# Three operations of an attention stage issued earlier in their step: the sum broadcast on TensorE, its copy on ScalarE, the main normalisation on VectorE

## The reference

```python
scores = q @ k.T / 8
scores = where(scores >= max(scores) - tau, scores, -1e9)
attn = exp(scores - max(scores)); attn /= attn.sum() + 1e-9
x = attn @ v                          # 2304 tokens x 512
h = relu(x @ w_in); x = (h * h) @ w_out
# then: 8 experts, each token goes to the best of x @ w_gate,
# relu(x @ w1[e]) @ w2[e], times its gate and a sigmoid
```

## Time and profile before

| | us |
|---|---|
| median of 3 runs | 1021.32 (1021.19 to 1021.54) |
| the profiled execution's own time | 1021.32 |
| its span, first to last instruction | 1019.6 |
| attention stage, of that | to about 317.6 |

### The profile page before, as it was taken

The page is one execution under the profiler, slowest core; times in us unless marked ns, Lnnn a source line. Parts: engine busy times, 40 slices in busy tenths (PEclk is TensorE's granted clock), DMA queues, the critical chain, the costliest instruction groups (busy, mean ns, idle before and its releaser), DMA issues.

```text
span 1019.6 us, 19281 instructions
## 1 busy us (share of the span) xinstructions
PE 994.8 (98%) x6731; PEld 828.7 (81%) x6731; DVE 627.0 (61%) x1220; ACT 585.8 (57%) x922; POOL 418.3 (41%) x725
## 2 busy tenths in 40 slices
PE   7999999999998999999999999999999999999996
PEld 5888888888886888888888888889978888888884
DVE  5888888888885334322322232235787777777773
ACT  4888787787774333322322232233548888888883
POOL 4777778778783000000000000000008866666763
PEclk9999999999999999999999999999999999999999
DMA  4322322322213110010011001005389157351110
GB/s 115 80 61 71 86 55 71 87 61 69 59 30 95 42 52 1 21 42 21 1 42 42 0 21 42 22 1 161 124 328 401 49 196 283 116 197 41 34 41 34
DMA packets 85385, 84.04 MB, mean 82 GB/s; under 512 B 49711, under 2 KB 64559, under 8 KB 85298
## 3 DMA queue, kind: packets, MB, share of 16 engines
q1 hardware_dynamic: 81778, 72.41, 23.9%
q0 software_dynamic: 3520, 10.49, 3.0%
HBM read 69.24 MB, written 15.21 MB: 83 GB/s over the span
## 4 chain that ended last, share of the span: by engine, by line
PE 66%; DVE 1%; SPq 0%; issue 0%; ACT 0%; DMA 0%; POOL 0%; ACTq 0%; POOLq 0%; DVEq 0%
PE y_ps L1167 19%; PE h_ps L1150 19%; PE y_ps L1231 16%; PE row_ps L1231 8%; PE h_ps L1262 2%; PE row_ps L1136 2%; PE y_ps L1221 1%; SPq L969 0%; SPq L965 0%; DMA y_rows<-r_buf 0%; DVE g_lo L1488 0%; ACT r_buf L1335 0%; PE h_ps L1136 0%; POOL out_dram L1058 0%; DVE y_row L1701 0%
## 5 line engine op out<-in xcount | busy, mean ns | idle before, releaser
L1483 DVE TENSOR_TENSOR g_buf<-r_buf 128x512 f32<-128x512 f32 (+1 forms) x80 | 51.1, 638 | 220.5 <-ACT r_buf L1335 219.8
L1335 ACT ACTIVATE r_buf<-h_ps 128x512 f32<-128x512 f32 (+1 forms) x80 | 44.4, 555 | 234.1 <-PE h_ps L1150 231.9
L951 POOL TENSOR_TENSOR w_lo<-w_experts,w_hi 128x2048 fp32r<-128x2048 f32 x20 | 126.2, 6309 | 73.9 <-ACT w_hi L1394 73.7
L1394 ACT ACTIVATE w_hi<-w_experts 128x2048 fp32r (+1 forms) x100 | 150.4, 1564 | 0.5 <-PE row_ps L1231 0.5
L1069 POOL MEMSET ones<- 128x128 bf16 x1 | 0.2, 210 | 356.9 <-DVE x_lo L1469 356.9
L477 ACT ACTIVATE e_sb<-s_sb,stats,live 128x576 f32<-128x576 f32 x144 | 124.5, 865 | 37.8 <-POOL stats L265 36.5
L951 DVE TENSOR_TENSOR w_lo<-w_experts,w_hi 128x1024 fp32r<-128x1024 f32 (+1 forms) x80 | 137.0, 1754 | 5.3 <-ACT w_hi L1394 5.0
L1150 PE MATMUL h_ps<-x_hi,w_in_hi 128*128 128x512 f32 (+1 forms) x320 | 119.9, 375 | 2.3 <-DVE x_lo L1469 2.3
L1167 PE MATMUL y_ps<-g_hi,w_out_hi 128*128 128x512 f32 (+1 forms) x320 | 118.0, 369 | 0.9 <-DVE g_lo L1488 0.9
L1150 PE MATMUL h_ps<-x_hi,w_in_lo 128*128 128x512 f32 (+1 forms) x320 | 117.9, 368 | 0.0
L1150 PE MATMUL h_ps<-x_lo,w_in_hi 128*128 128x512 f32 (+1 forms) x320 | 117.8, 368 | 0.0
(11 more groups left out here) (251 smaller groups left out, 2217.8 us busy)
## 6 DMA issues: line engine op xcount, KB each, us to landing
w_experts<-in_moe_w_dram SPq DMA_DIRECT2D x18, 2048.0 KB, 13.9
y_rows<-y_row SPq DMA_DIRECT2D x36, 128.0 KB, 2.4
k_raw<-in_k_dram SPq DMA_DIRECT2D x32, 128.0 KB, 3.1
q_raw<-in_q_dram SPq DMA_DIRECT2D x32, 128.0 KB, 2.9
w_raw<-in_moe_w_in_dram SPq DMA_DIRECT2D x16, 256.0 KB, 3.2
v_nat<-in_v_dram SPq DMA_DIRECT2D x16, 256.0 KB, 2.6
y_T<-in_moe_w_out_dram SPq DMA_DIRECT2D x16, 256.0 KB, 2.7
y_early<-y_row SPq DMA_DIRECT2D x32, 128.0 KB, 2.4
```

What stands on the lines that cost most here:

```text
L951: alu.tensor_tensor(group_of(w_lo, g)[:, c0:c1], raw_group(buf, g)[:, c0:c1], group_of(w_hi, g)[:, c0:c1].bitcast(F32), ALU.subtract).then ...
L1394: nc.scalar.activation(group_of(w_hi, g)[:, c0:c1], raw_group(buf, g)[:, c0:c1], ACT.Copy).then_inc(hi_done, 1)
L1483: V.tensor_tensor(g_buf[:, 0:cols], r_buf[:, 0:cols], r_buf[:, 0:cols], ALU.mult).then_inc(sq_done, 1)
```

## The change

Nothing is added or removed. In three loops a call is put further up in its step. On PE, in step `5i+1`, `broadcast_rinv(i-1)` comes ahead of the two sets of tail transposes of pair `i-1`. On ACT, in the same step, `copy_rinv(i-1)` comes ahead of their two copies. On DVE, in step `5i+2`, `normalise_main(i-1)` comes ahead of the two masks of step `5i+1`.

```diff
@@ block.tensor
+                if c == 1 and i >= 1:
+                    broadcast_rinv(i - 1)
                 if 0 <= made[0] < PAIRS:
                     for s in range(2):
                         transposed_probs(*made, s)
-                if c == 1 and i >= 1:
-                    broadcast_rinv(i - 1)
@@ block.scalar
+                if c == 1 and i >= 1:
+                    copy_rinv(i - 1)
                 if 0 <= made[0] < PAIRS:
                     for s in range(2):
                         evacuate(*made, s)
-                if c == 1 and i >= 1:
-                    copy_rinv(i - 1)
@@ block.vector
+                if c == 2 and i >= 1:
+                    normalise_main(i - 1)
                 if c == 3 and i >= 1:
                     normalise_tail(i - 1)
                 if 0 <= before[0] < PAIRS:
                     for h in heads_in(before[1]):
                         mask(*before, h)
-                if c == 2 and i >= 1:
-                    normalise_main(i - 1)
```

## The result

| | before | after |
|---|---|---|
| median of 4 runs, us | 1021.43 | 1029.14 |
| lowest to highest | 1021.19 to 1022.22 | 1028.88 to 1029.41 |
| profiled execution, its span | 1021.32, 1019.6 | 1030.98, 1029.3 |

The ratio is 1.0075, with a 95% interval of 1.0056 to 1.0092: slower by 7.7 us, against a forecast of 6.4.

A forecast was written before the change was run, and what follows sets the result against it. PE was taken to bound attention. Second-mask waits 4.40, broadcast waits 2.73 in short pairs and -0.28 in long ones, and the emptying -0.45 gave +6.40 us on 1021.32: 1027.7 us, range 1022.5 to 1031.5.

The forecast's parts named there:

- PE sets the pace, long and short pairs differ by one stall: Attention: PE's lateness is paid for; long pairs stall about 0.43 us in step 5i, behind ACT's copy.
- The mask's wait, 14 x 0.31: Step 5i+3: PE's second transpose set waits for DVE's later second mask; 4.40 us with 0.06 in the last pair.
- The broadcast's wait, 0.39 in short pairs: Step 5i+1: PE's broadcast waits for k's low part; 2.73 us over seven short pairs, -0.28 over seven long.
- The bound of 0.47: Upper limit for the short pairs' broadcast delay, if PE's release costs 0.08 more, as an accumulator read takes.
- The last pair waits for nothing at the broadcast: Pair 15 has no next k, so PE's moved broadcast has no wait there.
- ACT's order costs nothing: Step 5i+1: ACT does the same three operations, already waits 0.33 us for PE, ends equally behind it; 0.
- The emptying gains 0.45: Behind the last pair, the broadcast fills PE's idle gap before the last tail block; -0.45 us.
- The sum: Whole kernel: 4.40 + 2.73 - 0.28 - 0.45 = +6.40 us, 1027.7.
- The lost race with POOL: Rival: a POOL operation runs first and moves both masks by 0.25 us; 3.5 more, 1031.2; chance 0.15.
- The faster case: Rival: earlier POOL work lets ACT run ahead, long pairs' stall goes, masks meet PE; -3.5 us, 1017.9; chance 0.06.

The follow-up runs named there:

- e4_split: The kernel before, but POOL splits a pair's fourth weight piece behind the bias of step 5i+4 instead of ahead of it: 1017.16 us, ratio 0.9952.
- e2_normalise: The kernel before with only the change's DVE edit, the main normalisation ahead of the two masks: 1023.24 us, ratio 1.0010.
- e3_between: The kernel before with the broadcast between the two tail sets on PE and its copy between their copies on ACT: 1021.52 us, ratio 0.9994.
- e7_after_split: All three edits of the change plus POOL's fourth weight piece split behind the bias, against the kernel before: 1029.55 us, ratio 1.0070.
- e5_idle: The kernel before with the main normalisation moved to DVE's idle slot in step 5i+1, ahead of q's low part: 1018.73 us, ratio 0.9963.
- e1_broadcast: The kernel before with only the change's PE and ACT edits, DVE as before: 1025.08 us, ratio 1.0026.

## Why the prediction was right, and what was mis-sized

The direction, the mechanism and the range held. By its steps:

- *PE sets the pace, long and short pairs differ by one stall.* Right. The prediction named ACT's copy as what ends the stall; e4_split shows that it begins one engine further back, in POOL's weight piece.
- *The mask's wait, 14 x 0.31.* About right. Measured 0.33 from the six transposes (1.20 - 0.87) and 0.32 from e2_normalise (18.88 - 18.56). The 0.35 between the two sets was taken from rows of two kinds, 0.87 for six and 0.52 for three behind a stall; three right behind the scores take 0.55. In the last pair 0.08, forecast 0.06.
- *The broadcast's wait, 0.39 in short pairs.* Mis-sized. It is 0.47 to 0.48. I took the price of DVE's release from start-up, 0.05; here k's low part ends at 189.22 and the weight load starts at 189.34, 0.12 behind it, in all 14 pairs alike. That is 0.07 more, and 5.45 us where I had 5.37 from scores to k. It counts in every pair, 14 x 0.08 = 1.1 us of the sum, since a long pair too now takes 5.45, against 5.41 before: a loss of 0.04 instead of a gain. The bound of 0.47 was reached, but not for the reason given with it; the last section has what the trace shows.
- *The last pair waits for nothing at the broadcast.* Wrong by 0.24: it waits for the widened reciprocal. The weight load's gap is 0.41, of which 0.17 is usual; the matmul's is 0.17.

```profile
304.74 0.66 PE L406 MATMUL m_ps<-ident,rinv_wide 128*128 128x128 f32 x4 [0.17 <-DVE rinv_wide L586]
```

- *ACT's order costs nothing.* Nothing speaks against it: the order of e3_between cost nothing, and PE's two waits make up the whole loss. The change's own order of the copies was not run apart from PE's edit.
- *The emptying gains 0.45.* About right: 0.55, from the tail transposes' block to the last product (2.10 us, 321.55 to 323.65, against 2.65, 312.93 to 315.58). Most of attention's end is a chain of waits, and this one is only cover that happened to be free.
- *The sum.* The two waits in 14 pairs are 14 x (19.34 - 18.56) = 10.9. With the last pair and the emptying, 10.9 + 0.24 + 0.08 - 3.0 - 0.55 = 7.7. From the first of the 14 transposes of k (30.46 before, 30.85 after) to the first h matmul (319.39, 327.46) the traces have 288.93 and 296.61: 7.7. The forecast of 6.4 was 1.3 short, of which 1.1 is the broadcast's wait and 0.24 the last pair's; the rest cancels.
- *The lost race with POOL.* POOL lost it: its two operations took 0.65 and 0.69 us instead of 0.20 and 0.26, and the masks beside them kept their start and their 0.81.
- *The faster case.* The long pairs' stall did go, as it says. But PE's two new waits took more than that gives, 10.9 against 3.0.

## What to carry to other kernels

On an engine that sets the pace, an instruction that needs a late result belongs behind work that needs nothing; moving it ahead of five transposes, 0.50 us of such work (weight loads at 183.93 and 184.43 before), cost 0.48 us in each pair though nothing was added. A stall has a price only while nothing else is later: one edit's gain can be the same microseconds as another's, so prices of halves (3.2 and 1.3) do not add up to the whole (7.7), nor do gains (e7_after_split). Before an operation is moved ahead on a busy engine, look for a place where that engine waits for another: there the normalisation cost nothing (e5_idle).

## What the runs showed of the hardware

**A wait in an instruction of its own.** The broadcast waits for two things. In the trace the weight load itself carries the wait for `wide_ready`, and the wait for `klo_done` stands in an instruction of its own just ahead of it, once in each of the 14 pairs (the q in PEldq marks the engine's sequencer, 51 is its duration in ns, and 34.5 and 286.0 are the first and last start):

```profile
L400 PEldq EVENT_SEMAPHORE  x14: 51/51/51, 34.5 to 286.0; - x14
```

The weight load starts 0.12 us behind the end of k's low part, which this separate wait is for. Where the last thing to come is what the instruction itself waits for, it starts 0.05 or 0.06 behind: at start-up behind k's low part (16.03 to 16.08), in the last pair behind the widened reciprocal (304.69 to 304.74), behind a mask's accumulator read (197.20 to 197.26). The 0.051 us of the separate instruction fits the difference, but no run exchanged the two waits, so this is read from the rows and not tested.

**The granted clock behind a wait of PE.** Between attention and the feed-forward stage PE waits 2.3 us in every profile here. In those of the kernel before, of e2_normalise and of e4_split the granted clock stayed at 1.00 behind it. In those of the change, of e1_broadcast and of five others it fell there to 0.50, the level of 1.2 GHz, with matmuls 0.43 us apart instead of 0.23: for about 7 us in the change (shares of 0.68 and 0.63 in two stretches of 5 us), for about half of that in e5_idle. In e3_between it fell one wait earlier as well, behind 1.64 us of idle time in the last pair:

```profile
311.17 0.52 PE L370 MATMUL t_ps<-ident,probs 128*128 128x128 f32 x3 [1.64 <-ACT probs_T L497]
```

A wait as long, 1.63 us, was followed by no fall in the profile of before. It differs between executions of one kernel too: of the 27 runs of the kernel before, the five with a mean granted clock of 0.993 or 0.994 took 1023.08 to 1023.55 us, and the three with 0.998 took 1020.44 to 1021.49. In the profiles it takes up to 2 us, so single profiles of this kernel can't be compared at their ends to better than that. What decides it stays open.
